# Chunked attention woven into a feed-forward product: the pieces of each head-block pair gathered into two slots, and scores that begin with a 64x64 tile

## The chip, the cores and the metric

The kernel runs on one core of a Trainium2 chip. The metric is the device time of one execution in microseconds (us). Before the change it was 1676.81 us, the median of three runs (1674.45 to 1678.32).

## The reference, cut to what matters

Attention is taken within chunks of 64 positions, for 8 batches and 8 heads of width 64; its rows are normalised and go through two feed-forward networks.

```
q_c = q.reshape(B, H, nc, chunk, D)            # chunk = 64, nc = 9
scores = scale * np.matmul(q_c, k_c.transpose(0, 1, 2, 4, 3))
attn = softmax(scores)                         # over the 64 keys of the chunk
out = np.matmul(attn, v_c)
x = out.transpose(0, 2, 1, 3).reshape(4608, 512)
xn = x / sqrt(mean(x * x) + 1e-6) * rms_g
x = (silu(xn @ w_gate) * (xn @ w_val)) @ w_out     # inner width 1536
h = x @ w_in
out = (h * clip(h + 3, 0, 6) / 6) @ w_out2         # inner width 2048
```

## The kernel before, in words

**The four engines and two queues.** The program is written out by hand: PE (TensorE), DVE (VectorE), ACT (ScalarE), POOL (GpSimd) and SP (whose instructions issue nearly all DMAs) each have their own instruction stream, in the order in which the code emits it, and they meet only at semaphores. An instruction that waits holds up everything behind it on its engine.

**The big products.** Each feed-forward product is a seven-product block scheme (o = 0 to 6), every product done in three passes (lines 934, 935, 936: high by high, high by low, low by high part of fp32r operands) over two kt. The first network's up products run over m = 0 to 35. One m has 14 slots (o = 0 to 6, two streams st: gate into `bx`, value into `by`); one slot is one `up_product`, six matmuls of 128x384. Slots are counted here through the whole program: slot number 14 m + slot.

**The attention.** It is done in 36 pairs n (two batches, one chunk, 8 heads: 128 rows). Pairs 0 to 5, and the scores of pair 6, come ahead of the products. The others are woven into m = 0 to 14: behind the product of a slot, PE does one of the pair's four pieces:

- SC, `scores(n)`, line 858: 16 matmuls of 64x64 tiles. The first of them (h = 0, c = 0) spans 128 output rows (`rows_of` gives it `slice(0, P)`), the other 15 span 64. Each fp32 matmul leaves two records in the trace, so a piece has 32.
- TR, `transpose_probs(n)`, line 881: 4 transposes of 128x128.
- AT, `attend(n)`, line 900: again 16 matmuls, the first with 128 rows.
- XX, `transpose_x(n)`, line 909: 4 transposes of 128x128.

`EARLY` gives the slots of (SC, TR, AT, XX) for pairs 6 to 17; from pair 18 on SC is at slot 7n - 56, and TR, AT, XX stand 5, 8 and 13 slots behind. So there is one pair to seven slots. Between the pieces stands a chain over the other engines, and each of its links has its place by slot too:

- behind SC: `shift_scores(n)` on DVE one slot later (line 1418 row maximum, line 1420 subtraction), `exponentials(n)` on ACT two slots later (line 1071); then TR.
- behind TR: `copy_probsT(n)` on ACT one slot later (line 1078); then AT.
- behind AT: `scale_attention(n)` on DVE one slot later (lines 1425, 1427, 1431), `mean_square(n)` on ACT two slots later (line 1085), `inverse_rms(n)` on POOL three later (line 1767), `norm_rows(n)` on ACT four later (line 1090); then XX.
- behind XX: `evict_x(n)` on DVE one slot later (line 1448). AT of the next pair waits for it, since it uses the same bank.

**Loads of the pairs.** SP loads q and k for two pairs at a time, in 16 DMAs (line 532), into `qk_a` or `qk_c`. The first of them waits until DVE has transposed the q and k that were in the buffer, and the slots of the loads of pairs 10 and 11 (from slot 5), 12 and 13 (from slot 19) and two more are fixed in `QK_FIRST`. DVE transposes them into `qkT` (`transpose_qk(n + 1)`, line 1408), 3 slots behind SC of pair n, or as many as `AFTER` says. v is in a single buffer `v_a`, loaded by SP one slot behind each AT (line 563). Two transposes count one pair.

**Also in those slots**: ACT copies (`snap`, line 1130) and DVE sums (`combine`, line 1479) of the products, the gate (lines 1156, 1495, 1500), the splitting of the next block's x and weights into high and low parts (lines 1105, 1115 on ACT, 1454, 1467 on DVE), sums on POOL, stores of h and x by SP (lines 571 to 642).

Of the kernel before, what the change touches and what calls it, by code (L numbers as in the profile page):

```python
# [10 lines left out]
P = 128  # L11
# [3 lines left out]
def chunked_attention_then_two_ffns(nc: bass.Bass, q, k, v, w_gate, w_val, w_out, rms_g, w_in2, w_out2, out):  # L15
# [27 lines left out]
    CH = 64  # L43
# [4 lines left out]
    NN = NSB * NG  # L48
# [116 lines left out]
    def c21_of(m, st):  # L165
        return 5 if m < B0 else 6 + st
# [13 lines left out]
    def bank(m, st, role):  # L180
        i = (m + {"a": 0, "c": 1, "b": 1}[role]) % 2
        if m < D0:
            return (bx, by)[st][:, i, 0:N]
        return (bx[:, i], by[:, i], att[:, AB + 1 - i])[st][:, 0:256]
# [81 lines left out]
    def prod_no(m, o, st):  # L266
        return 14 * m + 2 * o + st + 1 if m < D0 else 14 * D0 + 3 * NO * (m - D0) + 3 * o + st + 1
# [7 lines left out]
    def comb_no(m, which, st):  # L275
        return 6 * m + which + st if m < D0 else 6 * D0 + 9 * (m - D0) + 3 * (which // 2) + st + 1
# [21 lines left out]
    def stores_of(m, st, apart):  # L298

        a_steps = B0 if st == 1 else 0  # L300
        if m < B0:
            return (m // 2 if apart else m) + 1
        return (a_steps // 2 + (m - C0) // 2 if apart else a_steps + m - C0) + 1

    def t_no(m, which, st=0):

        place = (1, 2, 4, 3).index(which)
        return 4 * m + place + 1 if m < B0 else 4 * B0 + 8 * (m - C0) + 2 * place + st + 1
# [122 lines left out]


    S_FIRST = NG
    EARLY = {6: (-6, -3, 1, 7), 7: (0, 3, 8, 12), 8: (7, 9, 14, 20), 9: (12, 15, 21, 24), 10: (18, 23, 26, 31), 11: (24, 28, 33, 37), 12: (32, 37, 39, 44), 13: (38, 43, 48, 51), 14: (46, 49, 52, 58), 15: (51, 53, 59, 64), 16: (57, 61, 66, 73), 17: (64, 66, 75, 77)}
    AFTER = {7: 5, 8: 1, 11: 5, 12: 5, 14: 1, 16: 5, 17: 5}
    SC, TR, AT, XX = 0, 1, 2, 3

    def at_slot_of(n, piece):
        return EARLY[n][piece] if n in EARLY else 7 * n - 53 - min(3, (n - 12) // 2) + (0, 5, 8, 13)[piece]

    def next_transposed_after(n):

        return AFTER.get(n, 3)

    WOVEN = range(S_FIRST, NN)

    def woven(m, slot, piece, after=0):

        for n in WOVEN:
            if at_slot_of(n, piece) + after == 14 * m + slot:  # L450
                return n
        return None
# [28 lines left out]
    for u in range(UB, U_B + 1):  # L481

        m = 20 + 3 * ((u - UB) // 2) if u % 2 == 0 else 21 + 3 * ((u - UB - 1) // 2)
# [342 lines left out]
    def score_bank(n):  # L826
        return bx[:, 0:2] if n < NG and n % 2 == 1 else att[:, SB:SB + 2]


    def rows_at(n):  # L830
        return xn_b if n < NG and n % 2 == 1 else xn
# [5 lines left out]
    def attended(n):  # L837
        return att[:, AB:AB + 2]
# [3 lines left out]

    @block.tensor
    def _(pe):
        def rows_of(h, c):
            return slice(0, P) if h == 0 and c == 0 else slice(c * CH, (c + 1) * CH)

        def scores(n):
            pe.wait_ge(q_transposed, n + 1)
            pe.wait_ge(k_transposed, n + 1)  # L850
            if n > 1:
                pe.wait_ge(probsT_copied, n - 1 if n <= NG else n)
            for h in range(H):
                e, j = h % 2, h // 2
                for c in range(2):
                    rows = rows_of(h, c)
                    mi = c * HJ + j
                    mm = pe.matmul(score_bank(n)[rows, e, j * CH:(j + 1) * CH], qkT[e * CH:(e + 1) * CH, 0, mi * CH:mi * CH + rows.stop - rows.start],  # L858
                                   qkT[e * CH:(e + 1) * CH, 1, mi * CH:(mi + 1) * CH], start=True, stop=True)
            mm.then_inc(scores_done, 1)  # L860
# [147 lines left out]
        for m in range(B0):  # L1008
            ph, s, j = m // 18, m % 18 // 3, m % 3
            f = NSB * ph + s  # L1010
            for slot in range(14):
# [12 lines left out]
                n = woven(m, slot, AT)  # L1024
                if n is not None:
                    attend(n)
                n = woven(m, slot, SC)
                if n is not None:
                    scores(n)
                n = woven(m, slot, TR)  # L1030
                if n is not None:
                    transpose_probs(n)
                n = woven(m, slot, XX)
# [364 lines left out]
    def _(dve):  # L1398
        def by_parity(r):
            return r.rearrange("p (j e n) -> p e j n", j=HJ, e=2)  # L1400

        def transpose_qk(n):
            buf, first, q_there, k_there = qk_of(n)
            if n > 0:
                dve.wait_ge(scores_done, n)
            for i, there, done in ((0, q_there, q_transposed), (1, k_there, k_transposed)):
                dve.wait_ge(*there)
                dve.transpose(qkT[:, i, :], buf[:, i, first:first + D]).then_inc(done, 1)
# [13 lines left out]
        def scale_attention(n):  # L1422
            o = attended(n)[:, :, 0:HJ * (DH + 1)].rearrange("p e (j n) -> p e j n", j=HJ)
            dve.wait_ge(attn_done, n + 1)
            dve.tensor_scalar(row_sum[:, :, :], o[:, :, :, DH], EPS_SOFTMAX, None, ALU.add).then_inc(sum_done, 1)
            dve.wait_ge(sum_done, n + 1)
            dve.reciprocal(row_recip[:, :, :], row_sum[:, :, :]).then_inc(recip_done, 1)
            dve.wait_ge(recip_done, n + 1)
            if n > 1:
                dve.wait_ge(x_transposed, n - 1 if n <= NG else n)  # L1430
            dve.tensor_tensor(by_parity(rows_at(n)[:, 0:D]), o[:, :, :, 0:DH], row_recip[:, :, :].unsqueeze(3).to_broadcast([P, 2, HJ, DH]), ALU.mult).then_inc(attn_scaled, 1)
# [55 lines left out]
        def gated(m, which):  # L1487
            i = {H12: 0, H22: 1, H11: 2, H21: 3}[which]
            dve.wait_ge(silu_done, 4 * m + i + 1)
            if which == H21:  # L1490
                dve.wait_ge(prod, prod_no(m, 6, 1))
                if m > 0:
                    dve.wait_ge(st_b[1], 16 * stores_of(m - 1, 1, False))
                    dve.wait_ge(t_done, t_no(m - 1, 4))
                dve.tensor_tensor(vb[:, c21_of(m, 1)], bank(m, 1, "a"), gb[:, G21], ALU.mult).then_inc(h_done, 1)
            else:
                dve.wait_ge(comb, comb_no(m, (K12, K22, K11)[i], 1))
                buf = vb[:, (c12_of, c22_of, c11_of)[i](m, 1)]
                gate = gb[:, (G12, G22, G11)[i]] if m < 18 else att[:, i, 0:N]
                dve.tensor_tensor(buf, buf, gate, ALU.mult).then_inc(h_done, 1)  # L1500
# [53 lines left out]
        for m in range(B0):  # L1554
            ph, s, j = m // 18, m % 18 // 3, m % 3
            f = NSB * ph + s + 1
            for slot in range(14):
                n = woven(m, slot, XX, 1)
                if n is not None:
                    evict_x(n)  # L1560
                if m > 0 and slot == 0:
                    gated(m - 1, H21)
                if m > 0 and slot == 1:
                    gated(m - 1, H11)
                n = woven(m, slot, SC, 1)
                if n is not None and n + 1 < NN and next_transposed_after(n) == 1:
                    transpose_qk(n + 1)
                if n is not None:
                    shift_scores(n)
                n = woven(m, slot, AT, 1)  # L1570
                if n is not None:
                    scale_attention(n)
                if m > 0 and slot == 3:
                    gated(m - 1, H22)
                if m > 0 and slot == 4:
                    gated(m - 1, H12)
                for after in (3, 5):
                    n = woven(m, slot, SC, after)
                    if n is not None and n + 1 < NN and next_transposed_after(n) == after:
                        transpose_qk(n + 1)  # L1580
                if slot in (7, 8):
                    comb_a(m, K12, slot - 7)
                if slot in (9, 10):
                    comb_a(m, K22, slot - 9)
                if slot in (11, 12):
                    comb_a(m, K11, slot - 11)
                if m == 0 and slot in FIRST_LO:
                    fill_lo(0, FIRST_LO[slot])
                if j == 2 and f < 12 and filled_at(f, slot - 1) is not None:
                    fill_lo(f, filled_at(f, slot - 1))  # L1590
                if j == 0 and m > 0 and filled_at(f - 1, slot + 13) is not None:
                    fill_lo(f - 1, filled_at(f - 1, slot + 13))
                for u, part in parts_at(LO_AT, m, slot):
                    weight_lo(u, part)
                splits(m, slot)
                if m == B0 - 1 and slot in (11, 13):
                    half_lo(0, 0, 0, (11, 13).index(slot))

        for s in range(NSB):
            m = B0 + s  # L1600
# [46 lines left out]
        for s in range(NSB):  # L1647
            m = D0 + s
# [260 lines left out]
```

## Time and profile before

| | |
|---|---|
| median of 3 runs | 1676.81 us (1674.45 to 1678.32) |
| span of the profiled execution | 1675.8 us, 1.0 us under the median |
| PE busy | 1645.6 us, 98% of the span |
| DVE, ACT, POOL busy | 62%, 52%, 44% |
| shares of the chain that ended last | PE 85%, DVE 3%, DMA 3%, issue 3%, POOL 3%, SP's queue 2%, ACT 2% |

Times are read from the start of the span. A row of the timeline gives the start, the time to the end of the last of the merged instructions, engine, line, tile names, shape and count. PE's instructions overlap, so what a piece costs is read from the starts of its neighbours and not from its own length.

### The profile page before, as it was taken

How to read it: one execution, taken by the hardware profiler on the slowest of the kernel's cores; microseconds unless marked ns; L12 is line 12 of the kernel's file. 1: busy time of each engine (PE TensorE's matmuls, PEld its weight loads, DVE VectorE, ACT ScalarE, POOL GpSimd, SP SyncE). 2: the span in 40 equal slices, each digit the busy share in tenths (PEclk: the TensorE clock that was granted, in tenths of full speed). 3: DMA queues.
4: the chain of work that ended last, by engine and by line, in shares of the span. 5: the costliest groups of instructions: out<-in, count | busy, mean ns of one | idle time of the engine just before them, and what ended most of it. 6: DMA issues, size and time to landing. Idle time of an engine off the chain costs nothing.

```text
span 1675.8 us, 31535 instructions
## 1 busy us (share of the span) xinstructions
PE 1645.6 (98%) x12297; PEld 1603.2 (96%) x12297; DVE 1034.0 (62%) x1407; ACT 867.4 (52%) x1375; POOL 731.0 (44%) x686
## 2 busy tenths in 40 slices
PE   7899999999999999999999999999999999999999
PEld 6788999999999999999999999999999999999999
DVE  4877868868755555664455776665666764444443
ACT  4665656655544444554444665554655653433432
POOL 2543434438786665432120467777766610010010
PEclk9999999999999999999999999999999999999999
DMA  9576767636465655888997866647648976676664
GB/s 177 133 186 150 172 164 177 151 118 192 152 231 203 206 206 184 315 311 306 313 317 287 300 228 235 223 178 254 221 162 300 377 252 199 200 224 204 197 222 132
DMA packets 334692, 366.98 MB, mean 219 GB/s; under 512 B 185104, under 2 KB 300560, under 8 KB 331344
## 3 DMA queue, kind: packets, MB, share of 16 engines
q1 hardware_dynamic: 322976, 334.69, 63.1%
q0 software_dynamic: 7104, 28.84, 4.8%
q10 hardware_dynamic: 4464, 1.44, 0.5%
q8 instruction: 97, 1.59, 0.4%
q14 instruction: 51, 0.42, 0.1%
HBM read 200.80 MB, written 164.10 MB: 218 GB/s over the span
## 4 chain that ended last, share of the span: by engine, by line
PE 85%; DVE 3%; DMA 3%; issue 3%; POOL 3%; SPq 2%; ACT 2%; DVEq 0%; ACTq 0%; POOLq 0%
PE bx L934 13%; PE by L934 12%; PE bx L936 12%; PE bx L935 12%; PE by L936 12%; PE by L935 12%; PE att L936 2%; PE att L934 2%; PE att L935 2%; PE att L900 2%; PE att L858 1%; DMA hl_b<-h_scratch 1%; SPq L539 1%; PE att L909 1%; PE att L881 1%
## 5 line engine op out<-in xcount | busy, mean ns | idle before, releaser
L934 PE MATMUL bx<-tx,wr 128*128 128x384 f32 x840 | 288.2, 343 | 2.7 <-ACT gb L1130 2.0
L934 PE MATMUL by<-tx,wr 128*128 128x384 f32 x840 | 287.3, 342 | 0.8 <-DVE ub L1479 0.6
L936 PE MATMUL bx<-tx,wr 128*128 128x384 f32 x840 | 281.9, 336 | 0.0
L935 PE MATMUL bx<-tx,wr 128*128 128x384 f32 x840 | 281.8, 335 | 0.0
L936 PE MATMUL by<-tx,wr 128*128 128x384 f32 x840 | 281.6, 335 | 0.0
L935 PE MATMUL by<-tx,wr 128*128 128x384 f32 x840 | 281.4, 335 | 0.0
L1505 DVE TENSOR_TENSOR hl_d<-hl_d 128x1536 fp32r<-128x1536 f32 x84 | 147.8, 1790 | 121.1 <-ACT hl_d L1210 121.0
L1505 DVE TENSOR_TENSOR hl_b<-hl_b 128x1152 fp32r<-128x1152 f32 x84 | 115.7, 1389 | 113.1 <-ACT hl_b L1210 112.5
L1210 ACT ACTIVATE hl_d<-hl_d 128x1536 fp32r<-128x1536 f32 x84 | 122.7, 1483 | 98.8 <-DMA hl_d<-u_scratch 98.5
L934 PEld LDWEIGHTS bx<-tx,wr 128*128 128x128 f32 x840 | 158.5, 189 | 7.0 <-issue 3.5
L934 PEld LDWEIGHTS by<-tx,wr 128*128 128x128 f32 x840 | 158.0, 188 | 4.9 <-DVE ub L1479 1.8
L1778 POOL DMA_DIRECT2D out_dram<-od x66 | 34.4, 528 | 288.0 <-DVE od L1479 217.9
L935 PEld LDWEIGHTS bx<-tx,wr 128*128 128x128 f32 x840 | 158.7, 189 | 0.0
L936 PEld LDWEIGHTS bx<-tx,wr 128*128 128x128 f32 x840 | 158.4, 189 | 0.0
L935 PEld LDWEIGHTS by<-tx,wr 128*128 128x128 f32 x840 | 158.1, 188 | 0.0
L936 PEld LDWEIGHTS by<-tx,wr 128*128 128x128 f32 x840 | 158.1, 188 | 0.0
L1210 ACT ACTIVATE hl_b<-hl_b 128x1152 fp32r<-128x1152 f32 x84 | 97.5, 1166 | 84.1 <-DMA hl_b<-h_scratch 83.9
L1479 DVE TENSOR_TENSOR gb<-bx,gb 128x384 f32<-128x384 f32 x108 | 59.4, 550 | 65.4 <-PE bx L936 65.3
L1526 DVE SCALAR_TENSOR_TENSOR ub<-att,ub 128x384 f32<-128x384 f32 x144 | 78.5, 556 | 32.0 <-ACT att L1240 32.0
L934 PE MATMUL bx<-wr,hl_d 128*128 128x256 f32 x336 | 95.3, 284 | 1.4 <-issue 1.0
L1767 POOL TENSOR_TENSOR inv_rms<-mean_sq,minus_half 128x1 f32<-128x1 f32 x36 | 26.1, 726 | 160.7 <-ACT att L1085 136.1
L935 PE MATMUL att<-wr,hl_d 128*128 128x256 f32 x336 | 95.1, 283 | 0.0
(184 smaller groups left out, 4365.0 us busy)
## 6 DMA issues: line engine op xcount, KB each, us to landing
hl_d<-u_scratch SPq DMA_DIRECT2D x84, 768.0 KB, 4.6
hl_b<-h_scratch SPq DMA_DIRECT2D x84, 576.0 KB, 6.2
u_scratch<-ut SPq DMA_DIRECT2D x48, 576.0 KB, 3.7
h_scratch<-ht SPq DMA_DIRECT2D x36, 576.0 KB, 3.6
u_scratch<-ub SPq DMA_DIRECT2D x96, 192.0 KB, 3.1
u_scratch<-ub SPq DMA_DIRECT2D x48, 384.0 KB, 2.5
h_scratch<-vb SPq DMA_DIRECT2D x72, 192.0 KB, 3.4
h_scratch<-vb SPq DMA_DIRECT2D x36, 384.0 KB, 3.1
```

Of the source, the lines that this page charges most:

```text
L539: sp.dma_start(qk_first[c * CH:(c + 1) * CH, n, which, :].rearrange("t (h d) -> t h d", d=DH), src[2 * p + c, :, t * CH:(t + 1) * CH, :].r ...
L858: mm = pe.matmul(score_bank(n)[rows, e, j * CH:(j + 1) * CH], qkT[e * CH:(e + 1) * CH, 0, mi * CH:mi * CH + rows.stop - rows.start], qkT[e ...
L900: mm = pe.matmul(banks[rows, e, j * (DH + 1):(j + 1) * (DH + 1)], prT[e * CH:(e + 1) * CH, j, rows], vv[e * CH:(e + 1) * CH, c * HJ + j, : ...
L934: pe.matmul(dst, w_hi, m_hi, start=start, stop=False, skip_group_check=not opens)
L935: pe.matmul(dst, w_hi, m_lo, start=False, stop=False, skip_group_check=not opens)
L936: return pe.matmul(dst, w_lo, m_hi, start=False, stop=stop, skip_group_check=not opens)
L1210: act.activation(buf[:, HI], buf[:, LO].bitcast(F32), ACT.Copy).then_inc(hl_hi, 1)
L1479: dve.tensor_tensor(buf, bank(m, st, role), buf, ALU.add).then_inc(comb, 1)
L1505: dve.tensor_tensor(buf[:, LO], buf[:, LO].bitcast(F32), buf[:, HI].bitcast(F32), ALU.subtract).then_inc(hl_lo, 1)
L1526: dve.scalar_tensor_tensor(buf, relu_to(i), 1.0, buf, ALU.min, ALU.mult).then_inc(u_done, 1)
L1767: pool.tensor_tensor(inv_rms[:, :], mean_sq[:, :], minus_half[:, :], ALU.pow).then_inc(rms_done, 1)
L1778: pool.dma_start(dst, src).then_inc(out_stored[s % 2], 16)
```

## The change

Three things are changed. The table `EARLY` and the rule for later pairs now put AT of pair n and SC of pair n + 1 in the same slot, and XX of pair n and TR of pair n + 1 in the same slot: for pairs 18 and later TR, AT and XX stand 5, 7 and 12 slots behind SC. `AFTER` keeps only three of its entries. Scores that stand directly behind an attend (`behind_attention`) begin with a 64-row tile like the rest. On DVE, `scale_attention` is emitted ahead of `shift_scores` when both fall in one slot.

```
     S_FIRST = NG
-    EARLY = {6: (-6, -3, 1, 7), 7: (0, 3, 8, 12), 8: (7, 9, 14, 20), 9: (12, 15, 21, 24), 10: (18, 23, 26, 31), 11: (24, 28, 33, 37), 12: (32, 37, 39, 44), 13: (38, 43, 48, 51), 14: (46, 49, 52, 58), 15: (51, 53, 59, 64), 16: (57, 61, 66, 73), 17: (64, 66, 75, 77)}
-    AFTER = {7: 5, 8: 1, 11: 5, 12: 5, 14: 1, 16: 5, 17: 5}
+    EARLY = {6: (-6, -3, 1, 6), 7: (1, 6, 8, 12), 8: (8, 12, 14, 19), 9: (14, 19, 21, 25), 10: (21, 25, 27, 31), 11: (27, 31, 33, 37), 12: (33, 37, 39, 44), 13: (39, 44, 46, 50), 14: (46, 50, 52, 56), 15: (52, 56, 58, 62), 16: (58, 62, 64, 68), 17: (64, 68, 70, 75)}
+    AFTER = {7: 5, 8: 1, 14: 1}
...
-        return EARLY[n][piece] if n in EARLY else 7 * n - 53 - min(3, (n - 12) // 2) + (0, 5, 8, 13)[piece]
+        return EARLY[n][piece] if n in EARLY else 7 * n - 53 - min(3, (n - 12) // 2) + (0, 5, 7, 12)[piece]
...
-        def rows_of(h, c):
-            return slice(0, P) if h == 0 and c == 0 else slice(c * CH, (c + 1) * CH)
+        def rows_of(h, c, whole=True):
+            return slice(0, P) if whole and h == 0 and c == 0 else slice(c * CH, (c + 1) * CH)
 
         def scores(n):
+            behind_attention = S_FIRST < n < NN and at_slot_of(n, SC) == at_slot_of(n - 1, AT)
...
-                    rows = rows_of(h, c)
+                    rows = rows_of(h, c, not behind_attention)
...
+                n = woven(m, slot, AT, 1)
+                if n is not None:
+                    scale_attention(n)
                 n = woven(m, slot, SC, 1)
                 if n is not None and n + 1 < NN and next_transposed_after(n) == 1:
                     transpose_qk(n + 1)
                 if n is not None:
                     shift_scores(n)
-                n = woven(m, slot, AT, 1)
-                if n is not None:
-                    scale_attention(n)
```

**On PE, at the slots where pair 24 begins (m = 8).** The rows are those of PE before: SC of pair 24, one product, AT of pair 23.

```order
L858 MATMUL att<-qkT 128x64
L858 MATMUL att<-qkT 64x64 x15
L934 MATMUL by<-tx,wr 128x384
L935 MATMUL by<-tx,wr 128x384
L936 MATMUL by<-tx,wr 128x384
L934 MATMUL by<-tx,wr 128x384
L935 MATMUL by<-tx,wr 128x384
L936 MATMUL by<-tx,wr 128x384
L900 MATMUL att<-v_a,pr 128x65
L900 MATMUL att<-v_a,pr 64x65 x15
```

And with the change, where the lines are numbered one higher:

```order
L901 MATMUL att<-v_a,pr 128x65
L901 MATMUL att<-v_a,pr 64x65 x15
L859 MATMUL att<-qkT 64x64 x16
L935 MATMUL by<-tx,wr 128x384
L936 MATMUL by<-tx,wr 128x384
L937 MATMUL by<-tx,wr 128x384
```

The product that stood between the two is gone from there, AT comes first, and the scores have no matmul of 128 rows. This happens for the AT of pairs 6 to 34, 29 times; before the change no AT and SC share a slot.

**On DVE, at the transposes of pair 11's q and k (m = 1).** Their two instructions are those that read `qk_a`; SP's load of pairs 12 and 13 waits for them. `row_max` and `pr` are the shift of pair 10's scores, `row_sum`, `row_recip` and `xn` the scaling of pair 9, `gb` and `vb` sums of products, `xr_odd` the eviction of pair 8. Before:

```order
L1418 TENSOR_REDUCE row_max<-att 128x8 [waits scores_done]
L1420 TENSOR_TENSOR pr<-att,row_max 128x2x4x64 [waits max_done]
L1448 TENSOR_TENSOR xr_odd<-att,g_col 128x4x128 [waits x_transposed]
L1408 STREAM_TRANSPOSE qkT<-qk_a 128x512 [waits q_loaded_a,scores_done]
L1408 STREAM_TRANSPOSE qkT<-qk_a 128x512 [waits k_loaded_a]
L1479 TENSOR_TENSOR gb<-bx,gb 128x384 [waits snap,prod]
L1425 TENSOR_SCALAR row_sum<-att 128x8 [waits attn_done]
L1427 RECIPROCAL row_recip<-row_sum 128x8 [waits sum_done]
L1431 TENSOR_TENSOR xn<-att,row_recip 128x2x4x64 [waits x_transposed,recip_done]
```

With the change:

```order
L1449 TENSOR_TENSOR xr_odd<-att,g_col 128x4x128 [waits x_transposed]
L1480 TENSOR_TENSOR gb<-bx,gb 128x384 [waits snap,prod]
L1426 TENSOR_SCALAR row_sum<-att 128x8 [waits attn_done]
L1428 RECIPROCAL row_recip<-row_sum 128x8 [waits sum_done]
L1432 TENSOR_TENSOR xn<-att,row_recip 128x2x4x64 [waits x_transposed,recip_done]
L1419 TENSOR_REDUCE row_max<-att 128x8 [waits scores_done]
L1421 TENSOR_TENSOR pr<-att,row_max 128x2x4x64 [waits max_done]
L1480 TENSOR_TENSOR vb<-by,vb 128x384 [waits snap,prod]
L1480 TENSOR_TENSOR gb<-bx,gb 128x384 [waits snap,prod]
L1409 STREAM_TRANSPOSE qkT<-qk_a 128x512 [waits q_loaded_a,scores_done]
L1409 STREAM_TRANSPOSE qkT<-qk_a 128x512 [waits k_loaded_a]
```

The transposes stand three slots later (slot 24, before 21) and now behind AT of pair 9, its scaling and the shift of pair 10. SP's load that waits for them keeps its slot, 19, and what follows it in SP's stream is the same set of DMAs.

## Rows read from the trace of the kernel before

**Rows 1.** What PE waited for, 44 to 375 us: total, times, longest.
```profile
PE att L881 <- ACT pr L1071: 4.2, 2, 3.6
PE att L909 <- ACT xn L1090: 3.7, 3, 2.7
PE att L858 <- issue: 1.6, 1, 1.6
PE att L900 <- issue: 1.5, 2, 1.3
```

**Rows 2.** Timeline of PE around SC of pair 24 and AT of pair 23.
```profile
238.79 0.34 PE L936 MATMUL bx<-tx,wr 128*128 128x384 f32 x1
...
240.32 0.34 PE L935 MATMUL by<-tx,wr 128*128 128x384 f32 x1
...
241.01 0.34 PE L936 MATMUL by<-tx,wr 128*128 128x384 f32 x1
241.28 1.05 PE L900 MATMUL att<-v_a,pr 64*128 64x65 f32 x32
...
242.54 0.34 PE L935 MATMUL bx<-tx,wr 128*128 128x384 f32 x1
```

**Rows 3.** Groups by line and shape, 239.0 to 240.03 us: busy us, mean ns.
```profile
L858 PE MATMUL att<-qkT 64*64 64x64 f32 x30 | 0.7, 225 | 0.0
```

**Rows 4.** Timeline of PE, the products around TR and XX in one slot.
```profile
117.69 0.34 PE L936 MATMUL by<-tx,wr 128*128 128x384 f32 x1
...
118.91 0.34 PE L935 MATMUL bx<-tx,wr 128*128 128x384 f32 x1
```

**Rows 5.** Timeline of PE, the products around TR alone.
```profile
246.36 0.34 PE L936 MATMUL by<-tx,wr 128*128 128x384 f32 x1
...
247.15 0.33 PE L935 MATMUL bx<-tx,wr 128*128 128x384 f32 x1
```

**Rows 6.** Timeline of PE, the products around SC and XX in one slot.
```profile
165.02 0.34 PE L936 MATMUL bx<-tx,wr 128*128 128x384 f32 x1
...
166.94 0.34 PE L935 MATMUL by<-tx,wr 128*128 128x384 f32 x1
```

**Rows 7.** Timeline of DVE: shift, scaling and transposes around pair 7; transposes of pairs 9, 11.
```profile
57.73 0.68 DVE L1418 TENSOR_REDUCE row_max<-att 128x8 f32<-128x512 f32 x1
...
59.05 0.16 DVE L1425 TENSOR_SCALAR row_sum<-att 128x8 f32<-128x8 f32 x1
...
60.09 1.29 DVE L1408 STREAM_TRANSPOSE qkT<-qk_a 128x512 f32<-128x512 f32 x2
...
69.72 1.30 DVE L1408 STREAM_TRANSPOSE qkT<-qk_a 128x512 f32<-128x512 f32 x2
...
90.91 1.29 DVE L1408 STREAM_TRANSPOSE qkT<-qk_a 128x512 f32<-128x512 f32 x2
```

**Rows 8.** Timeline of SP's queue: first loads behind a wait, v, x store.
```profile
71.11 2.99 SPq L532 DMA_DIRECT2D qk_a<-in_q_dram  x6
...
92.28 0.86 SPq L532 DMA_DIRECT2D qk_a<-in_q_dram  x2
...
119.00 1.30 SPq L563 DMA_DIRECT2D v_a<-in_v_dram  x2
...
121.01 0.56 SPq L571 DMA_DIRECT2D x_scratch<-xr  x1
```

**Rows 9.** Timeline of PE: AT of pair 8.
```profile
80.70 1.02 PE L900 MATMUL att<-v_a,pr 64*128 64x65 f32 x32 [0.20 <-issue]
```

**Rows 10.** Timeline of POOL, then of ACT, ahead of XX of pair 12.
```profile
127.10 1.85 POOL L1718 TENSOR_TENSOR xr<-xr 128x768 f32<-128x768 f32 x1 [3.65 <-DMA x_scratch<-xr]
...
132.31 0.72 ACT L1090 ACTIVATE xn<-xn,inv_rms 128x512 f32<-128x512 f32 x1 [2.41 <-POOL inv_rms L1767]
```

**Rows 11.** Windows: busy of PE, PEld, DVE, ACT, POOL, then granted clock, DMA.
```profile
60.00:66.00 6.00, 6.00 (x21) 6.00 (x22) 5.63 (x6) 5.97 (x12) 3.20 (x3) 0.50 0.01 3
...
240.00:330.00 90.00, 90.00 (x976) 82.89 (x971) 72.43 (x123) 58.55 (x107) 39.90 (x32) 1.00 0.68 166
```

## The prediction

> **What bounds the kernel now.** I read the page first: PE is busy 98% of the span and 85% of the chain that ended last lies on it. So an edit pays only if it takes time out of PE's own stream or takes away one of its waits. Then the waits of PE over the woven part [rows 1]: the three to read are TR waiting for the exponentials (4.2 us, twice), XX waiting for the normed rows (3.7 us, three times), and SC and AT waiting on something the profile calls issue (3.1 us); with small ones about 11 us in some 320. The rest of that stretch is matmuls one behind the other, so the next view is the timeline of PE around a piece, where the reader is to see from start to start and not by lengths. Products follow each other every 0.173 us (240.32 to 241.01 is four steps) [rows 2]. A granted clock by windows [rows 11] shows one stretch at 0.50, 60 to 66 us, behind the longest wait; from 240 to 330 us it is 1.00 and PE has no idle time at all.
>
> **What a piece costs PE.** From the last product matmul ahead of SC to the second one behind it are 240.32 - 238.79 = 1.53 us; two normal steps would be 0.35, so SC costs 1.18. AT: 242.54 - 241.01 gives the same 1.18 [rows 2]. TR alone: 0.79 - 0.35 = 0.44 [rows 5]. XX I take as TR: same shape, same count. One pair is therefore 3.24 us of PE beside its seven products.
>
> **Part 1, AT and SC in one slot, SC with 64-row tiles only.** Within SC the 30 records of 64*64 shape are busy 0.7 us together, of which about 0.2 is the length of the last one [rows 3], so each adds 16 ns and 32 of them 0.5 us. The other 0.68 us of SC's 1.18 is handover: into another tile shape, through a first matmul of a third shape, and back. Behind AT with the same 64x64 tile none of that should be paid again. A merge then saves 1.18 - 0.50 = 0.68 us. Both bounds: with a perfect joint it could be 0.72 (the last 0.04 being the rounding of the row); from below I take what SC and XX in one slot save today, where the shape does change between them: 1.92 - 0.35 = 1.57 against 1.18 + 0.44 = 1.62, that is 0.05 us [rows 6]. The new place is nearer to the inside of a piece than to that row, so 0.68. 29 merges are 19.7 us.
>
> The Trainium skill, TensorEngine Tiling (Array Packing), section Tiling Modes, says that the array drains when the tiling mode changes, and not when only the tile does. By it the joint is free and the merge saves the whole handover; the rows inside SC agree, and no row here shows the joint itself.
>
> **Part 2, TR and XX in one slot.** There is one such slot already: 118.91 - 117.69 = 1.22, less 0.35 is 0.87 us, just twice 0.44 [rows 4, 5]. Gain 0. These pieces have the shape of the products around them, so there is nothing to hand over. The eight or so places where the old table put SC and XX, or AT and TR, in one slot give their 0.05 back: 0.4 us lost in all, 0.3 of it behind slot 44.
>
> **Part 3, what the moved slots do to the first pairs.** This is where I expect most of the gain to go. The order of events, with the durations of DVE's blocks from its timeline: shift 1.3 us (57.73 to 59.05), scaling 1.04, two transposes 1.3 [rows 7].
>
> - *Slots 1 to 8.* DVE is busy with the first block's x and weights until 57.7 and takes the shift of pair 7 then. It will take the scaling of pair 6 first, so the shift and TR of pair 7 come about 1.1 us later, at 61; but TR now stands in slot 6 with XX of pair 6, which waits for ACT until about 65. PE idles in slots 5 to 6 as long as it did in slot 3, and I let the clock fall to half as it did [rows 11]. AT of pair 7 and SC of pair 8 end near 71.2. Two merges' gain is gone there. The transposes of pair 9 follow the scaling of pair 7: 72 to 73.2, against 69.72 to 71.0. That is +2.
> - *The first blocked load.* SP waits for those transposes and starts the loads of pairs 10 and 11 at 71.11 [rows 8]; v of pair 8 is issued behind ten of them, and AT of pair 8, at 80.70, waits for it [rows 9]. So AT of pair 8 goes to 82.8, SC of pair 9 now follows it instead of being done earlier, and slot 15 begins at 84.4 (before at 80.70 + 1.0).
> - *The second blocked load.* AT of pair 9 ends seven products, a TR with XX and itself later: 84.4 + 7.3 + 0.9 + 1.1 = 93.7. Then on DVE scaling 1.04, shift 1.3, two sums 1.0, transposes of pair 11 1.3: done at 98.4. Before they stood ahead of that AT and were done at 92.2 [rows 7], and SP's loads of pairs 12 and 13 began at 92.28 [rows 8]. So +6.2.
> - *What hangs on it.* From 92.28 to the x store at 121.01, SP issues one DMA after another without a pause (45 of them), the same ones after the change. v of pair 12 (119.00) and the x store (121.01) therefore move by 6.2 whatever PE does [rows 8]. The store's landing releases POOL at 127.10, POOL delays the inverse root, and ACT norms pair 12 at 132.31 to 133.03, for which PE waits with XX in slot 44 [rows 10]. XX of pair 12 goes from 133.1 to 139.3.
>
> Seven merges lie ahead of that point and all that they save (4.8 us) is swallowed, with 6.2 us on top. Behind it lie 22 merges: 22 x 0.68 = 15.0.
>
> **Part 4, shorter distances.** From pair 13 on TR stands four or five slots behind SC, AT two behind TR (before three and more), XX four or five behind AT. The chain behind a merged slot is, from the end of AT: scaling 1.1, shift 1.4, exponentials 0.65, so 3.2 us when DVE and ACT are free; four products and the scores' 0.5 give 4.7. DVE is 80% busy from 240 to 330 us [rows 11], and its load comes denser by 7%. What queues behind a late shift are the sums that the products o = 5 and 6 wait for. I take 0.8 us of new waits in all; from nothing to 8 (0.3 for each later pair).
>
> **Sum.** -15.0 + 0.3 + 6.2 + 0.8 = -7.7 us. Made against the profiled execution (span 1675.8, 1.0 under the median of 1676.81), that is a span of 1668.1 and a time of 1669. A difference under 0.2%, 3.4 us, can't be told from no change.
>
> **The rivals.**
>
> 1. *The first pairs don't slip, and all merges pay* (0.21). If PE's idle time in slots 1 to 8 is less, since TR no longer stands in slot 3 (its wait of 3.6 is most of the 4.2 [rows 1]), DVE's transposes come as early as before and SP with them. Then -19.7 + 0.4 + 0.8 = -18.5, or 1658. Against it stands DVE's order: the transposes of pair 11 are behind AT of pair 9 now, whatever came before.
> 2. *The distances are too short* (0.12). Each of the 22 later pairs waits 0.3 us: 1669 + 6 = 1675 to 1677, no change to be told. For it: TR waits twice and XX three times already [rows 1]. Against: PE has no idle time from 240 to 330, with chains that will be about as long as the new distances allow.
> 3. *The slip is dearer than worked out* (0.10). PE stands still for 6 to 8 us in slot 33 before v and the evicted x come, and its clock falls to half as it did from 60 to 66 us. There 14 to 16 matmuls took twice their time, some 2.4 us; two such falls, and DVE's queue held by the late transposes, give +5 on the forecast: 1674. The Trainium skill, TensorE: Matmul & The Clock Gate, states that idle time puts the array back to half rate; rows 11 agree with it.
> 4. *The joint is not free* (0.10), the slower side. If SC behind AT pays a handover as SC before XX does, a merge saves 0.05: 22 x 0.05 = 1.1, and the slip stays: -1.1 + 0.3 + 6.2 + 0.8 = +6.2, or 1683. It decides against the change when a merge saves less than (0.3 + 6.2 + 0.8) / 22 = 0.33 us. Only rows 6 speak for it, and there the shape does change.
>
> **How the numbers follow.** The forecast has 0.47: 1669, with its own range 1664 to 1673. The range 1657 to 1677 takes in rival 1 and rivals 2 and 3 and leaves out rival 4 and some of the far side of rival 1. Faster by over 3.4 us: the forecast, rival 1, most of rival 3: 0.76. Within: rival 2, a little of 3: 0.12. Slower: rival 4 and what is left: 0.12.
>
> **What would show it.** In the timeline of PE, the distance across a merged slot should be 2.0 us (1.53 + 0.5), 1.7 over two normal steps; across TR with XX 1.22 as today. SP's loads of pairs 12 and 13 should start near 98, AT of pair 11 near 120, XX of pair 12 near 139. From there on PE should gain 0.68 us a pair, and m = 15 start about 8 us earlier; behind m = 15 nothing should change. A distance of 2.6 us across a merge proves rival 4; SP's second load at 92 proves rival 1; waits of TR, AT or XX at most pairs prove rival 2.

## The result, and the profile after

The change made the kernel slower. The changed kernel takes 1691.55 us in the median (1687.52 to 1696.85, 4 runs), the kernel before took 1677.57 us on the same chip (1674.45 to 1679.13, 4 runs): a ratio of 1.0079, with a 95% interval of 1.0052 to 1.0107. (The ratios here are estimates over all the runs; these two medians divide to 1.0083.) The forecast of 1669 us and its range are missed, and by the slower side. The profiled execution has a span of 1690.1 us.

**Where it goes.** I lay the two timelines of PE over each other and take, for each m, the start of the first product in the changed kernel minus the one before. The first product of m = 3 starts 10.0 us later than before, that of m = 5 15.8 us later, m = 16 8.0 us, and the last stage of all, the down products of the second network, 14.3 us. So there are four stretches: a loss of 10.0 up to m = 3, 5.8 more up to m = 5, a gain of 7.8 up to m = 16, and 6.3 lost behind m = 16, where the change moves nothing in the program.

**The merged slot** is as forecast. Timeline of PE in the changed kernel; the answer to [rows 2]:

```profile
303.12 0.34 PE L937 MATMUL by<-tx,wr 128*128 128x384 f32 x1
303.39 0.99 PE L901 MATMUL att<-v_a,pr 64*128 64x65 f32 x29
...
304.23 0.68 PE L859 MATMUL att<-qkT 64*64 64x64 f32 x31
...
305.12 0.34 PE L936 MATMUL bx<-tx,wr 128*128 128x384 f32 x1
```

305.12 - 303.12 is 2.00 us, less two steps 1.65, where AT and SC apart cost 1.18 each: a merge saves 0.71 us (0.68 was forecast), and 1.65 us is the median over all 29 slots.

**What PE waits for** has grown, though, from some 11 us to 35. Waits of PE from 44 to 375 us in the changed kernel, total, times, longest; the answer to [rows 1]:

```profile
PE att L910 <- ACT xn L1091: 11.4, 10, 3.3
PE att L901 <- issue: 7.1, 2, 6.7
PE att L901 <- DMA v_a<-in_v_dram: 4.1, 1, 4.1
PE att L882 <- ACT pr L1072: 2.6, 2, 1.6
PE att L901 <- DVE xr_odd L1449: 1.9, 2, 1.0
PE bx L935 <- ACT gb L1162: 1.9, 1, 1.9
```

The wait for the exponentials shrank from 4.2 to 2.6. The norm (L1091) makes XX wait ten times instead of three, and attends now wait for v and for the evicted x (L1449). The two longest, in PE's timeline (the number in brackets is the idle time ahead and what ended it), are AT of pair 8, in answer to [rows 9], and AT of pair 10:

```profile
82.52 1.62 PE L901 MATMUL att<-v_a,pr 64*128 64x65 f32 x29 [4.10 <-DMA v_a<-in_v_dram]
...
111.70 1.61 PE L901 MATMUL att<-v_a,pr 64*128 64x65 f32 x29 [6.67 <-issue]
```

"issue" names nobody. SP's queue does; its timeline, in answer to [rows 8]:

```profile
72.35 2.99 SPq L532 DMA_DIRECT2D qk_a<-in_q_dram  x6
...
101.96 0.86 SPq L532 DMA_DIRECT2D qk_a<-in_q_dram  x2
102.87 0.49 SPq L632 DMA_DIRECT2D h_scratch<-vb  x1
103.40 1.23 SPq L532 DMA_DIRECT2D qk_a<-in_q_dram  x2
104.68 0.57 SPq L571 DMA_DIRECT2D x_scratch<-xr_odd  x1
105.29 1.69 SPq L532 DMA_DIRECT2D qk_a<-in_q_dram  x2
107.02 1.34 SPq L563 DMA_DIRECT2D v_a<-in_v_dram  x2
...
131.36 0.56 SPq L571 DMA_DIRECT2D x_scratch<-xr  x1
```

The load of pairs 12 and 13 starts at 101.96, 9.7 us later than before, and v of pair 10 is issued at 107.02, behind it. Its data are in place at 111.6, and AT of pair 10 starts. Why the load starts so late stands in DVE's timeline; its last row here answers to [rows 7]:

```profile
97.30 0.17 DVE L1426 TENSOR_SCALAR row_sum<-att 128x8 f32<-128x8 f32 x1 [1.49 <-PE att L901]
...
98.34 0.68 DVE L1419 TENSOR_REDUCE row_max<-att 128x8 f32<-128x512 f32 x1
...
100.13 0.55 DVE L1480 TENSOR_TENSOR gb<-bx,gb 128x384 f32<-128x384 f32 x1
100.59 1.29 DVE L1409 STREAM_TRANSPOSE qkT<-qk_a 128x512 f32<-128x512 f32 x2
```

The transposes stand behind AT of pair 9 (96.19), its scaling and a shift, and end at 101.9. So: AT of pair 9, DVE, SP's load, v, AT of pair 10, one behind the other. In the windows at and behind both waits the granted clock is low. Windows in the changed kernel, columns as in [rows 11] (busy of PE, PEld, DVE, ACT, POOL, then granted clock, DMA):

```profile
82.00:86.00 4.00, 3.48 (x67) 3.28 (x68) 1.63 (x4) 0.00 (x0) 1.75 (x3) 0.54 0.59 93
...
110.00:114.00 4.00, 2.30 (x64) 2.21 (x64) 0.45 (x3) 0.00 (x0) 0.00 (x0) 0.50 0.91 192
114.00:118.00 4.00, 4.00 (x26) 3.88 (x20) 2.98 (x5) 1.39 (x4) 0.23 (x1) 0.70 0.81 195
...
240.00:330.00 90.00, 88.31 (x1018) 83.59 (x1018) 68.08 (x126) 57.00 (x105) 38.99 (x34) 1.00 0.71 171
```

At 0.50 the array runs at 1.2 GHz instead of 2.4: a product matmul follows the last one after 0.32 us and not 0.173. From 44 to 375 us 26 steps were that long, 22 before. XX of pair 12, at 133.1 before, starts at 145.36 [rows 10].

**The waits that stay.** From 240 to 330 PE was busy all of the time before [rows 11]; now it lacks 1.7 us. An XX late for its norm, PE and then ACT:

```profile
279.52 0.60 PE L882 MATMUL att<-ident,pr 128*128 128x128 f32 x4
280.83 0.66 PE L910 MATMUL att<-ident,xn 128*128 128x128 f32 x4 [0.72 <-ACT xn L1091]
```

```profile
276.75 1.28 ACT L1072 ACT_TABLE_LOAD   x1
278.05 0.63 ACT L1072 ACTIVATE pr<-pr 128x512 f32<-128x512 f32 x1
278.59 0.83 ACT L1106 ACTIVATE tx<-xr 128x768 fp32r<-128x768 f32 x1
279.32 0.47 ACT L1131 ACTIVATE gb<-bx 128x384 f32<-128x384 f32 x1
279.69 0.48 ACT L1131 ACTIVATE vb<-by 128x384 f32<-128x384 f32 x1
280.06 0.72 ACT L1091 ACTIVATE xn<-xn,inv_rms 128x512 f32<-128x512 f32 x1
```

TR is in time and XX behind it in the same slot isn't: ACT has a table load of 1.28 us, the exponentials, a split of x and two copies to do ahead of the norm, without a gap. TR with XX costs 1.82 here instead of 0.88; over the whole table its median is 1.09. At every sixth of the later pairs AT waits too, about 1.0 us for the evicted x, and the merged slot of AT and SC then costs 2.69 and not 1.65.

### The profile page after: what moved, and what is told of

Its sections match the earlier page's. It is cut to its first block, busy times and chain, and to the rows that moved or that the text cites. A ratio compares the mean times of both kernels' runs of the same rounds, so it can differ in the third digit from the quotient of the medians.

```text
span 1690.1 us, 31537 instructions
## 1 busy us (share of the span) xinstructions
PE 1634.8 (97%) x12297; PEld 1598.8 (95%) x12297; DVE 1026.3 (61%) x1407; ACT 869.0 (51%) x1377; POOL 724.1 (43%) x686
## 4 chain that ended last, share of the span: by engine, by line
PE 81%; DMA 4%; issue 4%; ACT 3%; DVE 3%; SPq 2%; POOL 2%; DVEq 0%; ACTq 0%; POOLq 0%
PE bx L935 12%; PE by L935 12%; PE by L937 12%; PE by L936 12%; PE bx L936 12%; PE bx L937 11%; PE att L936 2%; PE att L937 2%; PE att L935 2%; DMA hl_b<-h_scratch 2%; PE att L901 2%; SPq L539 1%; PE att L910 1%; PE att L859 1%; DVE tx L1455 1%
## 5 line engine op out<-in xcount | busy, mean ns | idle before, releaser
L1131 ACT ACTIVATE gb<-bx 128x384 f32<-128x384 f32 x108 | 52.8, 489 | 89.1 <-PE bx L937 50.7
L935 PE MATMUL bx<-wr,hl_d 128*128 128x256 f32 x336 | 95.3, 284 | 1.3 <-issue 1.0
L937 PE MATMUL bx<-wr,hl_d 128*128 128x256 f32 x336 | 95.2, 283 | 0.0
```

The source lines that it names most:

```text
L935: pe.matmul(dst, w_hi, m_hi, start=start, stop=False, skip_group_check=not opens)
L937: return pe.matmul(dst, w_lo, m_hi, start=False, stop=stop, skip_group_check=not opens)
L1131: act.activation(dst, bank(m, st, role), ACT.Copy).then_inc(snap, 1)
```

## The experiments

Two theories to begin with. **Theory 1**: the loss is made by the slots of the first pairs, and the merges from pair 18 on pay. **Theory 2**: the shorter distances take back what the merges pay, everywhere. "Offset" is always the start of the first product of an m minus that of the kernel before, in the profiled executions. Between executions with the same slots up to m = 5 it varied (-3.1 in late_only, -0.4 in late_xx13, +4.5 in square_sooner), so the ratios decide. Part of that is the clock: from 44 to 190 us the granted clock was 0.99 in the profile of late_only and 0.96 in those of late_xx13 and of the kernel before.

**late_only.** The old slots and `AFTER` for pairs 6 to 17, the new spacing for the rest. Two entries of the old table move a little, so that pair 17 meets pair 18:

```
-16: (57, 61, 66, 73), 17: (64, 66, 75, 77)
+16: (57, 61, 66, 72), 17: (64, 66, 73, 76)
```

> Pairs 6 to 15 keep the slots of the kernel before, pairs 16 and 17 are moved by one or two slots to join on, and only from pair 18 on the changed table holds (AT with SC, XX with TR, 17 merges). Theory 1, the loss comes from the first pairs, through SP's blocked loads, and the later merges gain: PE stands at the first kernel's place at pair 17 and gains about 0.37 us a pair as in the changed kernel, so about 6 us under the kernel before, 1671. Theory 2, the shorter distances of the later pairs lose as much as the merges save or more: no gain, 1677 or above. On either, XX of pair 12 stays near 133 us.

1671.68 us, ratio 0.9974 (0.9959 to 0.9988) to before. Offset -3.1 at m = 5, -8.6 at m = 16. The profiled execution was a fast one: 8.9 us under that of the kernel before, where the ratio says 4.4.

**early_only.** The other half: the new slots for pairs 6 to 17, then the old spacing.

```
-(0, 5, 7, 12)[piece]
+(0, 5, 8, 13)[piece]
```

> The changed table for pairs 6 to 17 (12 merges), the old distances from pair 18 on. Theory 1 (the loss is in the first pairs): at m = 5 PE is 15 us behind the kernel before, and with nothing to win it back the time is 1691 to 1697, above the changed kernel without its chance waits. Theory 2 (the later pairs lose): at most 1683.

1693.02 us, ratio 1.0105 (1.0086 to 1.0124). Offset +10.1 at m = 3, +17.4 at m = 5, and 15.8 from m = 8 to m = 16 without a change. Theory 1 stands, Theory 2 falls: the early half costs at least as much as the whole change (the intervals overlap), the late half gains. With the old distances from pair 18 on PE has no wait at all from 190 to 375 us here; in the changed kernel it has 5.1 us of them there, so the new distances do make the waits.

**whole_first.** The changed slots, but the scores behind an attend keep their first matmul of 128 rows.

```
-rows = rows_of(h, c, not behind_attention)
+rows = rows_of(h, c)
```

> The changed kernel, but the scores behind an attend begin with the 128-row matmul again. Inside SC the two records of that matmul take 0.36 us before the next starts. If the change of shape is paid each time, the distance across a merged slot grows from 1.65 us by 0.3 to 0.4 to about 2.0, and at pairs where PE does not wait elsewhere all of it shows: 29 x 0.35 = 10 us at most, 5 to 10 likely, near 1698. If the shape of the first matmul is of no account, the time is that of the changed kernel, 1691, and the distance 1.65.

1700.34 us, ratio 1.0143 (1.0114 to 1.0172). The merged slot in its timeline:

```profile
303.70 0.34 PE L937 MATMUL bx<-tx,wr 128*128 128x384 f32 x1
303.97 1.05 PE L901 MATMUL att<-v_a,pr 64*128 64x65 f32 x32
304.95 1.05 PE L859 MATMUL att<-qkT 64*128 64x64 f32 x32
...
306.21 0.34 PE L936 MATMUL by<-tx,wr 128*128 128x384 f32 x1
```

306.21 - 303.70 is 2.51, or 2.16 over two steps (about 2.0 was expected): with the 128-row matmul a merge saves 0.20 us, and the 64-row tile the other 0.51. No run gives the scores their 64-row tile without the merge, so how much of the 0.51 could be had without moving a slot stays open. From m = 8 to m = 14 this kernel loses 1.6 us: 0.20 a pair is less than the waits of the new spacing.

**late_xx13.** As late_only, and XX 13 slots behind SC, in a slot without TR. Only AT and SC are still merged.

```
-(0, 5, 7, 12)[piece]
+(0, 5, 7, 13)[piece]
```

> As late_only, but XX stays 13 slots behind SC, so that only AT and SC are merged; the transposes have a slot each, as before. In the changed kernel XX of every second pair waited about 0.95 us for the normed rows, and TR with XX in one slot had cost no less than two slots. If that wait is what keeps the late gain at half of 0.68 us a merge, this kernel gains 0.65 or so for each of 17 pairs: 11 us under the kernel before, 1666. If the wait is made up elsewhere (DVE or ACT the bound of the stretch), it is the same as late_only, 1671.

1668.73 us, ratio 0.9952 (0.9936 to 0.9968): the fastest of all, and faster than both the kernel before and the changed one. It is 3.0 us under late_only by the medians of 12 runs each, on the same chip; 1666 and 0.65 us a pair were expected. XX no longer waits. Waits of PE from 190 to 375 us, of late_only and then of late_xx13:

```profile
PE att L910 <- ACT xn L1091: 2.4, 4, 0.7
PE att L901 <- DVE xr_odd L1449: 1.8, 2, 1.0
PE att L901 <- DVE xr L1449: 1.0, 1, 1.0
```

```profile
PE att L901 <- DVE xr_odd L1449: 2.7, 4, 1.2
PE bx L935 <- DVE tx L1455: 1.0, 3, 0.3
PE att L901 <- DVE xr L1449: 1.0, 2, 0.8
```

Some of the wait is at AT, which needs the evicted x one product after XX: a pair gains 0.39 us from m = 8 to m = 14 (4.65 / 12), against 0.30 in late_only.

**square_sooner.** As late_only, with the mean square on ACT one slot sooner.

```
-                n = woven(m, slot, AT, 2)
+                n = woven(m, slot, AT, 1)
                 if n is not None:
                     mean_square(n)
```

> The kernel late_only (1671.7) with mean_square one slot behind AT on ACT instead of two, so that it does not stand behind a copy that waits for the next product. In late_only and in the changed kernel XX waits for the normed rows at every second or third pair, 0.2 to 0.95 us, and the norm stands on ACT behind squares, table load and exponentials. If the late place of the squares on ACT is what delays the norm, XX's waits from pair 18 on go and the time falls by 2 to 3 us to 1669. If it is the table load and the exponentials ahead of the norm, the waits stay and so does the time.

1677.23 us, ratio 0.9994 (0.9976 to 1.0012). From m = 5 to m = 16 its offset falls by 7.9 us (from +4.5 to -3.4), late_only's by 5.5, but its profile was 4.5 us late at m = 5, where late_only was 3.1 early, and 7 us above the median. That lateness is TR waiting for the exponentials, 10.5 us from 44 to 190 us against 4.2 in late_only; whether the edit made it or this execution isn't known. XX's waits from 190 to 375 us shrank from 2.4 us (four times) to 1.7 (twice) and didn't go, and the times show no gain. So the late place of the squares is at most a part of it.

Then the early loss. **v_first**: v of pair 10 goes ahead of the load that waits.

```
-    QK_FIRST = {5: (5, 2), 6: (19, 2), 7: (26, 2), 8: (41, 2)}
+    QK_FIRST = {5: (5, 2), 6: (23, 2), 7: (26, 2), 8: (41, 2)}
```

> The changed kernel with the loads of pairs 12 and 13 four slots later in SP's stream (from slot 23), so that v of pair 10 is issued ahead of the load that waits for DVE. In the changed kernel AT of pair 10 stood 6.7 us for that v. Theory A (v behind the blocked load makes the loss itself): AT of pair 10 does not wait, m = 2 begins 7 to 8 us earlier than in the changed kernel and some 5 us of it last to the end, about 1686. Theory B (SP's stream of 45 DMAs from the transposes of pair 11 on sets the pace whatever PE does): the wait at AT of pair 10 goes, but PE stands at AT of pairs 11 and 12 or XX of pair 12 instead, XX of pair 12 moves by 2 us at most and the time is 1690.

1698.9 us, ratio 1.0103 (1.0076 to 1.0131). v is issued at 98.51 and AT of pair 10 starts at 106.18 without a wait, yet the offset is +15.3 at m = 3. The interval overlaps that of the changed kernel; against turn11_sooner and both_loads below, on the same chip, it is 6 to 7 us slower. The load that was pushed back meets the next one, and SP issues the two in turns. DVE's timeline, then PE's:

```profile
111.99 0.71 DVE L1409 STREAM_TRANSPOSE qkT<-qk_a 128x512 f32<-128x512 f32 x1 [1.17 <-DMA qk_a<-in_q_dram]
122.51 0.71 DVE L1409 STREAM_TRANSPOSE qkT<-qk_a 128x512 f32<-128x512 f32 x1 [9.81 <-DMA qk_a<-in_k_dram]
```

```profile
124.85 1.11 PE L910 MATMUL att<-ident,xn 128*128 128x128 f32 x4 [10.25 <-ACT xn L1091]
```

The wait of 6.7 us is gone, and one of 10.25 stands in its place, at XX of pair 10: DVE is held by the late k, and ACT behind DVE. Neither theory's time (1686, 1690) came.

**turn11_sooner**: the transposes of pair 11 one slot behind SC of pair 10.

```
-    AFTER = {7: 5, 8: 1, 14: 1}
+    AFTER = {7: 5, 8: 1, 10: 1, 14: 1}
```

> The changed kernel with the transposes of pair 11 one slot behind SC of pair 10 instead of three, ahead of its shift on DVE. SP's blocked load then starts about 2.5 us sooner (99.5 instead of 101.9). If the loss hangs on the moment when that load is let go, everything up to XX of pair 12 comes 2 to 2.5 us sooner and the time is 1689; if not, it stays at 1691.

1692.91 us, ratio 1.0070 (1.0046 to 1.0095). SP's load starts at 98.26, 3.7 us sooner, AT of pair 10 waits 3.3 instead of 6.7, the offset at m = 3 is +6.4. But at m = 5 it is +15.0. **both_loads** has this edit and v ahead of the load (`6: (22, 2)`):

> Both of these edits, with the loads from slot 22. Theory A: v of pair 10 is on time and SP is let go sooner, the two gains add up, 1684. Theory B: the second alone counts, 1688.

1691.94 us, ratio 1.0068 (1.0044 to 1.0092); +8.9 at m = 3 and +17.7 at m = 5. AT of pair 10 doesn't wait here either, and XX waits 5.9 us instead; neither 1684 nor 1688 came, and neither edit gains clear of the noise. Whatever was won at m = 3 was gone at m = 5, so I looked for a second loss there. The last three kernels look for it.

**slots_to_12** has the new slots for pairs 6 to 12 and from 18 on, and the old ones for 13 to 17. **slots_from_13** has the old ones for 6 to 12 and the new ones from 13 on. In the first, pairs 16 and 17 join on as in late_only. `AFTER` goes with the slots: the first keeps the old entries of 16 and 17, the second those of 11 and 12.

```
slots_to_12:    12: (33, 37, 39, 44), 13: (38, 43, 48, 51), 14: (46, 49, 52, 58)
slots_from_13:  12: (32, 37, 39, 44), 13: (39, 44, 46, 50), 14: (46, 50, 52, 56)
```

> The changed kernel with the slots of before for pairs 13 to 17; pairs 6 to 12 and the later ones as changed. It tells which part of the early loss the two loads behind waits make up. The changed kernel stood 10.0 us behind before at the start of m = 3, 15.8 at m = 5 and 8.0 at m = 16. Theory A (two separate losses: the late loads of pairs 12 and 13, and then too short distances at pairs 13 to 17): here m = 3 stands at +10 and m = 5 still at +8 to +11, m = 16 at +3 to +5, a ratio near 1.003 to 1.005. Theory B (one loss, which goes on: the late load alone makes what follows late): m = 5 at +14 to +16 and the ratio that of the changed kernel, 1.007 or 1.008.

> The other half: pairs 6 to 12 in the slots of before, pairs 13 and on as changed. Theory A (two losses): m = 3 at 0 (within 1.5), m = 5 at +3 to +6, m = 16 at -4 to 0, a ratio of 0.998 to 1.001. Theory B (only the late loads cost): m = 5 at -3 as in the kernel with the changed slots from pair 18 on alone, m = 16 at -8 or below, a ratio of 0.996 or less.

| kernel | ratio to before | offset m = 3 | m = 5 | m = 16 |
|---|---|---|---|---|
| late_only | 0.9974 (0.9959 to 0.9988) | -1.4 | -3.1 | -8.6 |
| slots_to_12 | 1.0009 (0.9999 to 1.0018) | +8.7 | +5.0 | -0.4 |
| slots_from_13 | 0.9991 (0.9973 to 1.0008) | +0.9 | +5.5 | -1.6 |
| changed kernel | 1.0079 (1.0052 to 1.0107) | +10.0 | +15.8 | +8.0 |

Two losses, then, each seen by itself. The ratio of slots_to_12 is clear of that of late_only; that of slots_from_13 is not (the intervals overlap), and there the waits and the offset at m = 5 speak. In slots_from_13 all numbers lie where the theory of two losses put them; in slots_to_12 they lie below both theories (m = 5 at +8 to +11 and a ratio of 1.003 to 1.005 were expected of this one), so the late loads cost less by themselves than I thought. What each half costs isn't settled. By the ratios the first slots cost 5.9 us, those of pairs 13 to 17 2.8, and both together 17.6, more than the sum by an amount just outside the noise. The offsets at m = 5 give 8.1, 8.6 and 18.9 against late_only, but that execution was a fast one; against late_xx13, with the same slots up to there, they give 5.4, 5.8 and 16.2. So a part of the loss seems to come only when the loads are late and the distances short, and why is open. No run undoes the new `AFTER` entries, or the new order on DVE, by itself.

In slots_to_12 the offset even falls from m = 3 to m = 5. Waits of PE from 120 to 190 us, slots_to_12 and then slots_from_13:

```profile
PE att L910 <- ACT xn L1091: 0.5, 1, 0.5
```

```profile
PE att L910 <- ACT xn L1091: 4.6, 4, 1.6
PE att L901 <- issue: 2.6, 1, 2.6
PE att L882 <- ACT pr L1072: 1.6, 1, 1.6
PE att L901 <- ACT pr L1079: 1.4, 2, 1.2
```

Pairs 13 to 17 wait at the new distances, with loads as early as before, and hardly at the old ones, though the loads came as late there as in the changed kernel (the one of pairs 12 and 13 from 100.62, the blocked one behind it from 136.18, against 101.96 and 136.17).

**after_xx13**: the changed kernel with XX 13 slots behind SC.

> The changed kernel with XX 13 slots behind SC instead of 12 for pairs 18 and later, so that XX stands in a slot alone and has one product more ahead of it. With the slots of before up to pair 17 this gained 2.9 us (1668.7 against 1671.7). If the norm that XX waits for at every second pair is what the short distance costs, it gains the same here: m = 5 unchanged (+15.8), m = 16 at +5 in place of +8, a ratio of 1.005 to 1.007. If that gain was of the chip job and not of the edit, it is the 1.008 of the changed kernel.

1686.34 us, ratio 1.0043 (1.0029 to 1.0056). Offset +18.1 at m = 5 and +8.8 at m = 16: from there the late pairs gain 9.4 us in place of 7.8, and from m = 8 to m = 14 0.41 us a pair in place of 0.31, as the product more for XX would have it. But m = 5 wasn't at the +15.8 that was expected, and the offset at m = 16 isn't smaller: the whole difference between the two profiled executions (14.3 against 8.7 at the end) arises behind m = 16, where this one loses 0.9 us and that of the changed kernel 6.3. The ratio is better than expected for a reason that isn't the edit's, as far as these traces go.

## Why the prediction was wrong

The forecast was -7.7 us, the profiled executions differ by +14.3 up to the last stage. The error of 22.0 us by stretch, from the offsets (the forecast's waits are put behind m = 5):

| stretch | forecast | measured | error |
|---|---|---|---|
| to m = 3 | +6.2 | +10.0 | 3.8 |
| m = 3 to 5, 4 merges | -2.7 | +5.8 | 8.5 |
| m = 5 to 16, 18 merges | -12.3 + 1.1 = -11.2 | -7.8 | 3.4 |
| behind | 0 | +6.3 | 6.3 |

**Part 1 held.** "A merge then saves 1.18 - 0.50 = 0.68 us": it is 0.71, and rival 4 with its 0.05 falls. whole_first adds what the forecast could not know: the merge alone gives 0.20, the 64-row tile 0.51. What the Trainium skill says (TensorEngine Tiling (Array Packing), section Tiling Modes), that the array drains when the tiling mode changes, agrees with the free joint; that the 128-row matmul brings back 0.51 us of the 0.71 agrees too, since it is the one step of another shape in the scores. The drain itself is in no row.

**Part 2 held**: TR with XX costs 0.88 where nothing is late. But one slot for two pieces also means that XX has one product less ahead of it, and the forecast looked at its price on PE alone.

**Part 3 is the first failure: "v of pair 12 (119.00) and the x store (121.01) therefore move by 6.2 whatever PE does".** The chain was right and was stopped too early. I followed SP's second load down to the x store and passed over what stands between, v of pair 10. It made PE stand 6.7 us and run at half clock. The transposes themselves ended at 101.9 and not at 98.4, since AT of pair 9 began at 96.19 and not near 92.6. AT of pair 8 was not to blame: it began at 82.52, where 82.8 was forecast. But behind its wait of 4.1 us the granted clock was 0.54 and then 0.61, which the forecast had only for slots 1 to 8: that piece with SC behind it took 2.5 us, 11 product steps took 0.32 each, and XX of pair 8 waited for its norm on top. SP's stream did move as a block, by 9.7 us at its head and 10.4 at the x store (131.36). Yet the last link was another one. POOL had the inverse root of pair 12 done at 140.44, and ACT normed only at 144.59: two table loads (137.79 and 139.74) had put it back, and it then stood 1.54 us for DVE. XX of pair 12 slipped by 12.3 us, not by 6.2, and AT of pair 11 came at 123.73 instead of 120. Rival 3 had the mechanism ("PE stands still for 6 to 8 us", a second fall of the clock) at 0.10, but it put the stall in slot 33, one pair too late, and stopped at 1674. turn11_sooner shows the link from transposes to load to AT of pair 10: 3.7 us sooner at the one end is 3.4 us less waiting at the other. That chain made the stall; that it made the whole loss up to m = 3 isn't shown, since the kernels in which AT of pair 10 doesn't wait are no faster.

**Part 4 is the larger failure: "I take 0.8 us of new waits in all; from nothing to 8".** Rival 2, "waits of TR, AT or XX at most pairs", at 0.12, is what came here, though its 1675 to 1677 counted no more than 6 us for it. For pairs 13 to 17 the forecast gain of 2.7 became a loss of 5.8 between m = 3 and m = 5 (of 4.5 in slots_from_13, where the loads are on time), and for the later pairs a merge that saves 0.71 left 0.31 (3.75 us over 12 pairs, m = 8 to 14). The chain had been worked out with "3.2 us when DVE and ACT are free", and only as far as the exponentials that TR needs; the chain of XX (squares, inverse root, norm) and that of the evicted x were not summed at all. ACT isn't free either: I left out its table load of 1.28 us and the copies that stand ahead of the norm. The Trainium skill, ScalarE: Activation LUTs, section What ACT_TABLE_LOAD costs, gives 1283 ns for the load, with which the trace agrees, and a drain of 1.38 us on top, which it doesn't show: the exponentials start at 278.05, 0.02 us behind the end of the load that began at 276.75, and the row ahead of it ends 0.02 us before it. And PE having "no idle time from 240 to 330" spoke for slack only as long as the distances stayed as they were. late_xx13 shows XX's share: given one product more, it waits no longer, and a pair gains 0.39 us where late_only gains 0.30. Over six of the later pairs of the changed kernel TR with XX costs 0.21, 0.21 and 0.94 us more than 0.88, and AT's wait 1.04, together 2.40: the 0.40 a pair that is missing from the 0.71.

**The check "behind m = 15 nothing should change" failed** in the profiled execution: 6.3 us are lost behind m = 16. Waits of PE from 375 to 1100 us in the changed kernel:

```profile
PE bx L935 <- DVE hl_b L1506: 3.6, 3, 2.2
PE by L935 <- DVE vb L1480: 1.8, 1, 1.8
PE bx L935 <- ACT gb L1131: 1.2, 2, 0.9
```

Both kernels have the same instructions there. Behind 400 us PE stood 9.9 us in this execution and 5.6 in that of the kernel before, and behind the longest of the waits (2.2 us, at 771.7) the granted clock was 0.72 from 770 to 776, where it had stayed at 1.00 before: together some 6 us. The same stretch costs -1.9 us in late_xx13, -0.3 in early_only, +0.4 in late_only, +0.9 in after_xx13, +1.2 in whole_first, +1.3 in slots_from_13, +3.9 in slots_to_12 and +6.6 to +9.4 in both_loads, v_first, turn11_sooner and square_sooner. It doesn't go with the edits in any way that I could see. Whether a shift of the starting point makes these waits, or whether they vary from execution to execution, stays open; so some 6 of the 14.3 us between the profiled executions have no cause here, and whether the other executions lose them too isn't known.

## What to carry to other kernels

A merge that saves time on the full engine is worth its price only where the chain behind it has slack: work out that chain with everything that the other engines do in between, table loads and copies included, and look for an offset that keeps the merge and gives back the distance. When a wait in an in-order queue moves, walk the queue instruction by instruction and ask who waits for each, not only for the last one. And test such a table of slots by stretches: here the first pairs and the next ones each cost, together, it seems, more than one by one, and the steady part alone was a gain.

## What the runs showed of the hardware

A single matmul of 128 rows at the start of the scores' 64x64 tiles, behind an attend, costs 0.51 us (2.16 against 1.65), three quarters of what the 31 records of the scores in the merged row last together (0.68). A table load on ACT took 1.28 us, with 0.02 us to the rows on either side. In v_first one wait was taken away and the kernel was no faster (6.7 us gone, 10.25 come), since the load that was let wait was needed by a third engine.
